# First batch of a fused recurrence, routing and token-mixing kernel: order of the first gates, loads and one weight split

## The reference, cut to what matters

```
f = 1/(1+exp(-f_logit))
state = f[t]*state + k[t] (outer) v[t];   y[t] = q[t] @ state
```

```
logits = x @ w_gate;  q,k,v = x @ wq[e], x @ wk[e], x @ wv[e]
a = causal softmax(q k^T / 8);  out += w[token,e] * (a @ v @ wo[e])
```

## Time and profile before

| | us |
|---|---|
| median of 3 runs | 568.41 |
| lowest, highest | 567.17, 569.14 |
| the profiled execution's own time | 567.73 |
| span of its records | 566.0 |
| PE busy in the span | 537.9 (95%) |
| DVE, ACT, POOL busy | 370.4, 298.0, 132.1 |

### The profile page before, as it was taken

One profiled execution on the slowest core, in us unless ns is written; L12 is line 12 of the kernel. 1 busy time (PEld: TensorE's weight loads), 2 busy tenths in 40 slices (PEclk: granted clock), 3 DMA queues, 4 the chain that ended last, 5 costly groups with the idle time before them and its releaser, 6 DMA issues.

```text
span 566.0 us, 14104 instructions
## 1 busy us (share of the span) xinstructions
PE 537.9 (95%) x5996; PEld 507.5 (90%) x5996; DVE 370.4 (65%) x672; ACT 298.0 (53%) x599; POOL 132.1 (23%) x88
## 2 busy tenths in 40 slices
PE   0999999999999999999999999999999999999997
PEld 0789888898789997899977899999999999999997
DVE  2987887888888777865867677555236544562434
ACT  5759687665876558633578574224222433133311
POOL 2004055044510035100123357112211212022200
PEclk9999999999999999999999999999999999999999
DMA  8948003062210530004500000010001100020002
GB/s 288 345 132 307 2 29 86 3 238 79 78 31 3 182 128 2 1 3 136 203 1 2 1 1 2 0 57 30 0 1 43 42 1 1 14 71 1 1 1 83
DMA packets 17969, 37.24 MB, mean 66 GB/s; under 512 B 2160, under 2 KB 10608, under 8 KB 17392
## 3 DMA queue, kind: packets, MB, share of 16 engines
q1 hardware_dynamic: 17904, 36.32, 18.5%
HBM read 31.46 MB, written 4.72 MB: 64 GB/s over the span
## 4 chain that ended last, share of the span: by engine, by line
PE 78%; ACT 8%; DVE 7%; issue 2%; DMA 2%; POOL 1%; SPq 1%; DVEq 0%; POOLq 0%
PE bank L1253 18%; PE bank L1254 18%; PE bank L1255 18%; ACT prob L728 5%; PE bank L1400 4%; PE bank L1271 4%; PE bank L1463 4%; PE bank L1352 3%; PE bank L1316 3%; PE bank L1359 2%; PE bank L1339 2%; DMA OT<-w_theta 2%; ACT probT L769 1%; PE bank L1563 1%; DVE gate L875 1%
## 5 line engine op out<-in xcount | busy, mean ns | idle before, releaser
L1253 PE MATMUL bank<-z_h,wt_h 128*128 128x384 f32 x288 | 97.7, 339 | 0.0
L1254 PE MATMUL bank<-z_l,wt_h 128*128 128x384 f32 x288 | 97.4, 338 | 0.0
L1255 PE MATMUL bank<-z_h,wt_l 128*128 128x384 f32 x288 | 96.5, 335 | 0.0
L728 ACT ACTIVATE prob<-bank,nmax 128x384 f32<-128x384 f32 (+5 forms) x96 | 60.2, 637 | 20.7 <-DVE nmax L1121 20.7
L524 POOL TENSOR_TENSOR trig<-trig,x 128x768 f32<-128x768 f32 x18 | 33.5, 1864 | 149.5 <-ACT trig L634 92.6
L1121 DVE TENSOR_REDUCE nmax<-bank 128x1 f32<-128x384 f32 (+5 forms) x96 | 54.9, 616 | 9.9 <-PE bank L1406 5.2
L967 DVE TENSOR_SCALAR turns<-bank 128x384 int32<-128x384 f32 x22 | 12.2, 556 | 74.0 <-PE bank L1255 74.0
L1253 PEld LDWEIGHTS bank<-z_h,wt_h 128*128 128x128 f32 x288 | 54.0, 188 | 0.6 <-issue 0.3
L1254 PEld LDWEIGHTS bank<-z_l,wt_h 128*128 128x128 f32 x288 | 54.1, 188 | 0.0
L1255 PEld LDWEIGHTS bank<-z_h,wt_l 128*128 128x128 f32 x288 | 54.0, 188 | 0.0
L843 ACT CAST uT_h<-bank 128x384 fp32r<-128x384 f32 x24 | 11.5, 478 | 78.5 <-PE bank L1563 78.5
(11 more groups left out here) (177 smaller groups left out, 1397.7 us busy)
## 6 DMA issues: line engine op xcount, KB each, us to landing
V<-v SPq DMA_DIRECT2D x4, 1152.0 KB, 10.9
gate<-fT SPq DMA_DIRECT2D x12, 384.0 KB, 3.2
q<-qT SPq DMA_DIRECT2D x12, 384.0 KB, 5.8
k<-kT SPq DMA_DIRECT2D x12, 384.0 KB, 6.3
wt_raw<-w_tok SPq DMA_DIRECT2D x6, 768.0 KB, 8.4
out<-x SPq DMA_DIRECT2D x24, 192.0 KB, 1.9
gate<-fT SPq DMA_DIRECT2D x3, 512.0 KB, 4.8
q<-qT SPq DMA_DIRECT2D x3, 512.0 KB, 9.9
```

Source lines behind the costliest of these rows:

```text
L728: nc.scalar.activation(prob[:, m % 2, r, at], bank[r][:, at], ACT.Exp, bias=nmax[:, m, k:k + 1], accum_out=den[:, m // 2, which, e:e + 1]) ...
L1253: nc.tensor.matmul(o, a_h, b_h, start=start, stop=False)
L1254: nc.tensor.matmul(o, a_h, b_l, start=False, stop=False)
L1255: return nc.tensor.matmul(o, a_l, b_h, start=False, stop=stop)
```

## The change

It touches the first batch alone.

1. SP issues `woT` and `w_theta` ahead of q and k of part 0.
2. Values of batch 0 come in two transfers: chunks 0 and 1 (semaphore `v_first`), then chunks 2 to 5 (`v_in`). PE waits for the first before the first outputs, behind the first `turn_k` instead of ahead of it, and for the second at c = 2.
3. ACT's order becomes Exp 0, Exp 1, Ln 0, Ln 1, Exp 2; then shrink 0, grow 0, shrink 1, grow 1, and the copy of the weight product behind them, where grow 1 was behind the copy. Ln of part 2 moves behind the first `kTs` copy.
4. At c = 1 ACT runs one Exp of a 128x1 column into a new tile `loaded`, which nothing reads.
5. At c = 2 grow of part 2 moves from ahead of the copy of chunk 1's outputs to behind it.
6. POOL begins `wvg_l` when `judged` is up, where it waited for the last state (`s_ready` at 5).

```diff
@@ load_v(b), SP
-                sp.dma_start(V[:, :, :], v[b]).then_inc(v_in, 16)
+                if b < 1:
+                    sp.dma_start(V[:, 0:2, :], v[b][:, 0:2, :]).then_inc(v_first, 16)
+                    sp.dma_start(V[:, 2:NT, :], v[b][:, 2:NT, :]).then_inc(v_in, 16)
+                else:
+                    sp.dma_start(V[:, :, :], v[b]).then_inc(v_in, 16)
@@ SP
-            load_first_qk(0)
             sp.dma_start(staged(W_OT, 768), woT).then_inc(w_in[3], 16)
             sp.dma_start(staged(W_TH, 1152), w_theta).then_inc(w_in[3], 16)
+            load_first_qk(0)
             load_first_qk(1)
@@ POOL
-            pool.wait_ge(s_ready, NT - 1)
+            pool.wait_ge(judged, 1)
             lo(wvg_l[:, :, 0:256], wv_raw, wvg_h[:, :, 0:256], wvg_lo)
@@ ACT; exp_first and log_first are the bodies of the two loops before
+            exp_first(0)
+            exp_first(1)
+            log_first(0)
+            log_first(1)
+            exp_first(2)
             shrink_first(0)
             grow_first(0)
             shrink_first(1)
+            grow_first(1)
             act.wait_ge(wth_mm, 1)
             nc.scalar.copy(staged(W_OTH, 768, 2), bank[2][:, :].rearrange("p (a n) -> p a n", a=2)[:, :, 0:D]
                            ).then_inc(wth_copied, 1)
-            grow_first(1)
@@ ACT, recurrence_copies, behind the copy of kTs
+                        if it < 1 and c == 0:
+                            log_first(2)
                         if it < 1 and c == 2:
                             shrink_first(2)
-                            grow_first(2)
                         if c >= 1:
                             act.wait_ge(y_done, upto(it, NT, c))
                             nc.scalar.copy(xn[:, c - 1, :], ps(out_bank(c - 1))[:, 0:D]).then_inc(x_copied, 1)
                         if it < 1:
-                            if c == 3:
+                            if c == 2:
+                                grow_first(2)
+                            elif c == 1:
+                                act.wait_ge(consts, 13)
+                                nc.scalar.activation(loaded[:, :], halfpi[:, :], ACT.Exp)
+                            elif c == 3:
@@ PE
-                pe.wait_ge(v_in, upto(it, 16, 16))
...
                 turn_k(0)
                 if it < 1:
                     pe.wait_ge(wth_copied, 1)
+                    pe.wait_ge(v_first, 16)
+                else:
+                    pe.wait_ge(v_in, upto(it, 16, 16))
                 outputs(0)
...
                 for c in range(1, NT):
+                    if it < 1 and c == 2:
+                        pe.wait_ge(v_in, 16)
```

More of the change, by code:

```diff
@@ L278, in build @@
         warm = s1("warm", [P, 1])
+        loaded = s1("loaded", [P, 1])
         steep = s1("steep", [P, 1], I32)
@@ L327, in build @@
         slow_step, slow_turn, slow_pair = sem("slow_step"), sem("slow_turn"), sem("slow_pair")
-        v_in = sem("v_in")
+        v_in, v_first = sem("v_in"), sem("v_first")
         f_in, q_in, k_in = ([sem(f"{n}{p}") for p in range(PAIRS)] for n in ("f_in", "q_in", "k_in"))
@@ L649, in grow_first, with exp_first, log_first @@
                 decay_chunks(chunks_of(n))
-            for n in range(PARTS):
+            def exp_first(n):
                 act.wait_ge(clamped, n + 1)
                 nc.scalar.activation(gate[:, :, part(n)], gate[:, :, part(n)], ACT.Exp, scale=-1.0).then_inc(expf, 1)
-            for n in range(PARTS):
+            def log_first(n):
                 act.wait_ge(expf, n + 1)
                 nc.scalar.activation(gate[:, :, part(n)], gate[:, :, part(n)], ACT.Ln, bias=1.0).then_inc(logf, 1)
+            exp_first(0)
[3 more added lines that the diff above has]
+            exp_first(2)
             shrink_first(0)
```

## The result

The changed kernel takes 565.07 us (median of 6 runs, 564.85 to 565.78); the kernel before, timed beside it, 568.07 (6 runs, 567.17 to 569.14). The ratio is 0.9949, interval 0.9937 to 0.9962: faster by 2.9 us, 2.2 to 3.6. The profiled execution took 565.0, its span is 563.3; before they were 567.73 and 566.0. The forecast was 565.8 and a gain of 2.55.

What follows compares the result with a forecast made beforehand. PE bounds the kernel (78% of the chain), so gains in the first 45 us shift everything: DVE 2.26 earlier plus 0.3 at the value product, 2.55; 567.73-2.55 = 565.18, as a median 565.9, forecast 565.8, range 564.2 to 567.6.

Steps and rivals of the forecast that it cites:

- Two paths to the scores: Before chunk 0's scores, weight product and scaled k both arrive at 20.3 to 20.5; removing one alone gives 0.2.
- The weights: First loads: `w_theta` ahead of q and k lands 3.0 earlier, at 10.9; its product runs 11.05 to 17.5.
- Rival A: First loads: weights land late; past 11.3 the product ends behind k, at 12.6 the time is 566.8; chance 0.12.
- the sum's 6.45: Length in us assumed for the weight product's 12 matmuls on PE, 11.05 to 17.5.
- Ln of part 2: DVE reaches part 2's scans at 22.9 and waits until 23.26; added table switches otherwise hidden, costing 0.35.
- Rival B: ACT becomes the bound before k of part 2; with 3.5 us of lateness the median is 569.1; chance 0.05.
- The drain: On ACT, some 1380 ns added per table switch by the skill's page; the forecast's load row did not show it.
- DVE 2.26 earlier: After the wait for part 2's Ln, DVE runs 2.26 us earlier than before, no longer 2.6.
- the weight split: POOL's `wvg_l` runs 34.7 to 37.1 once `judged` is up; first value product gains 0.3, at most 0.38.
- Rival C: PE runs at half speed for some 4.6 us in the recurrence; median 570.5; chance 0.04.
- Rival D: Start earlier but not the end: PE's stages between 45 and 100 us absorb it; gain 0.5 to 1.5; chance 0.11.

Runs made afterwards that it cites:

- c_loads_only: The kernel before with only `woT` and `w_theta` loaded ahead of q and k of part 0; 568.17 us, ratio 1.0004 to the kernel before.
- d_gates_only: The changed kernel with `w_theta` loaded behind q and k of part 0 again; 567.36 us, ratio 0.9987 to the kernel before.
- k_again: Repeat: changed kernel with `wvg_l` made by DVE and the last gates' clamp moved behind weighing of the outputs; 565.21 us, ratio 0.9949.
- f_no_dummy: The changed kernel without the one-column Exp at c = 1; 565.78 us, ratio 0.9968 to the kernel before.
- changed_again: The changed kernel itself, unaltered, measured once more in another group; 565.40 us, ratio 0.9952 to the kernel before.
- a_split_late: The changed kernel with POOL waiting for the last state again before `wvg_l`; 565.48 us, ratio 0.9956 to the kernel before.

## Why the prediction was right

The time, the sign and the main mechanism were right, one step failed, and a part of the agreement in time is luck. The median of 565.07 lies just below the forecast's own range of 565.1 to 566.7 and within the wider one, 564.2 to 567.6.

- Two paths to the scores, taken away together: forecast 17.9, measured 18.14 and 18.35 (the second part of the gates was there 0.3 later than in the profile before). c_loads_only and d_gates_only show that neither edit does it alone.
- The weights: landing forecast at 10.9, first matmul at 11.03. The 12 matmuls took 5.55 instead of 6.45, and nothing hung on it. Rival A's limit of 11.3 was passed in eight of the twelve profiles with the loads ahead (11.0 to 11.8), and in seven of these PE still waited 0.85 to 3.00 for k, so the landing alone did not bring rival A about. In the eighth, k_again, whose rows stand behind this list, the product did set the start of the scores: k was ready at 17.94 there, and the scores came 0.58 behind it, where the changed kernel has 0.13. The same 12 matmuls took 5.50 to 7.13 in the twelve profiles, with weight loads 0.64 apart for the first 2.7 us in the changed kernel and for 5.9 in k_again, and a granted clock of 1.00 in both. So the sum's 6.45 was 0.9 too long for some executions and 0.7 too short for one, and there it is a part of rival A. What sets the length of the slow stretch stays open.
- Ln of part 2: a wait of 0.36 forecast, 0.17 measured; ACT's copies came where they were placed, within 0.5. f_no_dummy bears out how narrow it is: one 1.28 us load in front of shrink 2, and 0.65 us are on the path. Rival B needed 2.8 us of lateness. The drain that would have brought it about does not show: in the rows of f_no_dummy the load ends at 27.71 and Exp starts at 27.72.
- DVE 2.26 earlier by the forecast; 2.04 measured at `steep` (36.77 and 34.73). The missing 0.22 is less than the 0.32 by which the gates' second part came later (clamped at 6.66 instead of 6.34).
- The step that failed is the weight split: "34.7 to 37.1 ... I take 0.3 gained". It started at 40.33 and gained nothing. The prediction read the start at 42.41 as held by the last state and the clamps, and did not ask of the idle time ahead of it, put down to no one, what it was: 9.73 us between POOL's all-reduce and its first subtraction. The runs show a change of configuration there and the first subtraction 7.3 to 9.7 us behind it, with the semaphore moved or not.
- Its 0.3 was made up for by chance: the load of gates at 96 us, which cost PE 0.90 in the profile before and 0.16 in the one after. So of the medians' 3.0, 2.0 are shown at the first value product (2.3 with the gates' landing set equal), and the rest is within what this load spreads. That it is this load in the medians too is not shown, since only one execution of each run has a trace; by the ratios changed_again gained 2.7 and a_split_late 2.5.
- Rival C, a slow stretch in the recurrence, had no part: PE stood 1.57 us behind the product, four times what was forecast, and the scores' 32 matmuls took 2.06 as before. Rival D, the gain lost further on, neither: the tail was not longer.

PE in k_again, the product of the weights and the scores of chunk 0 without a wait between them:

```profile
11.46 7.13 PE L1318 MATMUL bank<-OT 128*128 128x384 f32 x12 [11.46 <-DMA OT<-w_theta]
18.52 2.06 PE L1288 MATMUL bank<-q,k 64*128 64x128 f32 x32
```

## What to carry to other kernels

Here two paths arrived within 0.2 us of each other, and neither edit alone could be told from none, while both together gave 2 us; count both before judging either. Idle time that the profile puts down to nothing is a cost with a cause: before a wait is moved, ask whether the wait was what ended it. A wait that keeps one engine out of another's way can be worth its time: here letting GpSimd go sooner cost VectorE 1.3 us, while giving the work to VectorE's own gap brought the first value product 0.4 to 0.5 forward.

## What the hardware showed that was not expected

- GpSimd's first plain subtraction behind its all-reduce came 8.1 to 9.7 us later, with a change of configuration at the start of that time; behind a plain copy, with the same change of configuration, 7.3.
- A clamp of 128x768 on VectorE, 0.61 us by itself, took 2.19 when it started beside GpSimd's subtraction of 1.92 (changed_again): four took 3.8 us instead of 2.2, in eight profiles.
- A load of 384 KB, issued alone, took 3.1 to 4.9 us to land in executions of nearly the same program. PE's wait behind it went from 0 to 1.43 us, and the span behind the first value product from 520.0 to 521.8.
- Twelve matmuls of the same weights took 5.50 to 7.13 us, with the granted clock at 1.00 (changed_again and k_again).
